# The masks' limits made two tiles at a time, and low parts moved ahead of them, in a fused attention and MLP kernel

## What is computed

```python
scores = scale * np.matmul(q, k.transpose(0, 1, 3, 2))        # 4 batches x 8 heads, 576 x 576, head_dim 64
thresh = np.max(scores, axis=-1, keepdims=True) - tau         # tau = 0.02
scores = np.where(scores >= thresh, scores, -1000000000.0)
attn = np.exp(scores - max); attn = attn / (sum + 1e-9); attn @ v
x = heads side by side                                        # 2304 tokens x 512
h = x @ w_in;  g = s * relu(h)**2 + b;  x = g @ w_out         # d_ff 2048
h = x @ w_in2; g = h * sigmoid(1.702 * h); out = g @ w_out2
```

## Time and profile before

| what | us |
|---|---|
| median of 3 runs (lowest to highest) | 1013.93 (1013.07 to 1015.03) |
| the profiled execution | 1013.14 |
| its span | 1011.3 |
| TensorE busy / VectorE busy | 988.5 (98%) / 796.9 (79%) |
| ScalarE / GpSimd busy | 606.3 (60%) / 658.3 (65%) |
| granted TensorE clock | full speed (1.00) throughout |

### The profile page before, as it was taken

One profiled execution on the slowest core, in us unless ns is written; L12 is line 12 of the kernel. 1 busy time (PEld: TensorE's weight loads), 2 busy tenths in 40 slices (PEclk: granted clock), 3 DMA queues, 4 the chain that ended last, 5 costly groups with the idle time before them and its releaser, 6 DMA issues.

```text
span 1011.3 us, 18111 instructions
## 1 busy us (share of the span) xinstructions
PE 988.5 (98%) x5872; PEld 890.6 (88%) x5872; DVE 796.9 (79%) x1747; ACT 606.3 (60%) x1124; POOL 658.3 (65%) x714
## 2 busy tenths in 40 slices
PE   5999999999999999999999999999999999999998
PEld 4888888888888888888899999998898989898897
DVE  6999999999999999999646765877667777556663
ACT  5887666666576666665545756554546545454453
POOL 5768997778888788887657775444534544445442
PEclk9999999999999999999999999999999999999999
DMA  6235776788777888678733441112122321222212
GB/s 205 82 99 168 204 207 208 193 242 237 211 192 196 225 218 222 191 185 214 207 122 126 172 162 34 41 64 84 42 84 71 118 84 43 83 82 106 84 47 78
DMA packets 97580, 142.48 MB, mean 141 GB/s; under 512 B 10320, under 2 KB 68944, under 8 KB 97488
## 3 DMA queue, kind: packets, MB, share of 16 engines
q1 hardware_dynamic: 97488, 141.34, 47.8%
HBM read 102.96 MB, written 4.72 MB: 106 GB/s over the span
## 4 chain that ended last, share of the span: by engine, by line
PE 87%; DVE 10%; issue 1%; ACT 1%; DMA 0%; POOL 0%; SPq 0%; DVEq 0%; POOLq 0%; ACTq 0%
PE shared L825 12%; PE y_ps L844 11%; PE shared L918 10%; PE y_ps L942 10%; PE scores L942 10%; PE scores L918 8%; PE scores L739 8%; PE scores L801 7%; PE scores L825 5%; PE y_ps L864 5%; DVE scores L1025 4%; DVE prob L1051 3%; PE scores L864 2%; DVE blocks L1065 1%; DVE limit L1032 1%
## 5 line engine op out<-in xcount | busy, mean ns | idle before, releaser
L1248 ACT ACTIVATE prob<-scores,neg_max 128x576 f32<-128x576 f32 (+1 forms) x160 | 118.6, 741 | 126.1 <-DVE scores L1025 124.0
L1590 POOL TENSOR_TENSOR a_sum_lo<-a_sum,a_hi 128x256 fp32r<-128x256 f32 x96 | 70.1, 740 | 182.7 <-DVE scores L1147 124.0
L1025 DVE TENSOR_SCALAR_CACHE_REDUCE scores<-scores,consts 128x576 f32<-128x576 f32 (+1 forms) x160 | 129.5, 809 | 18.1 <-PE scores L739 16.6
L1539 POOL TENSOR_TENSOR w_lo<-w_raw,win_hi 128x512 fp32r<-128x512 f32 x96 | 129.0, 1344 | 22.1 <-ACT win_hi L1290 17.7
L1546 POOL TENSOR_TENSOR w_lo<-w_raw,wout_hi 128x512 fp32r<-128x512 f32 x96 | 126.4, 1316 | 23.6 <-ACT wout_hi L1297 23.5
L1533 POOL TENSOR_SCALAR prob<-prob,row_inv 128x576 f32<-128x576 f32 (+1 forms) x160 | 126.5, 803 | 5.5 <-DVE row_inv L1039 5.0
L1051 DVE SCALAR_TENSOR_TENSOR prob<-scores,limit,prob 128x576 f32<-128x576 f32 (+1 forms) x160 | 128.1, 808 | 0.9 <-ACT act_hi L1258 0.9
L825 PE MATMUL shared<-act_hi,win_hi 128*128 128x384 f32 x280 | 94.9, 339 | 1.1 <-DVE gate L1081 0.9
L825 PE MATMUL shared<-act_hi,w_lo 128*128 128x384 f32 x280 | 94.4, 337 | 0.0
L739 PE MATMUL scores<-k_hi,q_hl 128*128 128x288 f32 (+1 forms) x320 | 78.0, 326 | 16.8 <-DVE prob L1051 9.0
L825 PE MATMUL shared<-act_lo,win_hi 128*128 128x384 f32 x280 | 94.0, 336 | 0.0
(11 more groups left out here) (154 smaller groups left out, 2945.1 us busy)
## 6 DMA issues: line engine op xcount, KB each, us to landing
w_raw<-slabs SPq DMA_DIRECT2D x93, 512.0 KB, 4.1
a_raw<-twin_in SPq DMA_DIRECT2D x24, 512.0 KB, 4.5
o_raw<-twin_out SPq DMA_DIRECT2D x24, 512.0 KB, 3.5
prob_t<-blocks SPq DMA_DIRECT2D x96, 120.0 KB, 2.7
k_raw<-k SPq DMA_DIRECT2D x32, 288.0 KB, 4.2
prob_t<-blocks SPq DMA_DIRECT2D x96, 96.0 KB, 2.9
v_sb<-v SPq DMA_DIRECT2D x26, 320.0 KB, 4.3
q_raw<-q SPq DMA_DIRECT2D x40, 192.0 KB, 4.4
```

What stands on the lines that cost most here:

```text
L1025: nc.vector.tensor_scalar(place, place, scale_c[0:m, :], None, ALU.mult, ALU.min, accum_out=neg_max[0:m, j % STATS:j % STATS + 1]).then_in ...
L1248: nc.scalar.activation(prob[0:m, j % PROBS, :].rearrange("p (a n) -> p a n", a=2), scores[j % 2][0:m, :, 0:HALF], ACT.Exp, bias=neg_max[0: ...
L1539: nc.gpsimd.tensor_tensor(in_of(w_lo, n), in_of(w_raw, n), win_hi[n % IN_HI][:].bitcast(F32), ALU.subtract).then_inc(win_lo_ready, 1)
```

## The change

The limits of both tiles of a beat become one instruction on two columns, which waits for both maxima (for `max_ready` at j + 2) and counts once for a pair, so that each mask waits for `limit_ready` at j // 2 + 1. It is issued after both maxima. The low part of the lone piece moves from between the two maxima to behind the second, and the low part of the gated slab from behind mask a to ahead of the limit.

```diff
-            def limit_of(j):
+            def limit_pair(j):
+
                 m, r = rows_of(j), j % STATS
-                dve.wait_ge(max_ready, j + 1)
-                nc.vector.tensor_scalar(limit[0:m, r:r + 1], neg_max[0:m, r:r + 1], tau_c[0:m, :], None, ALU.add
+                dve.wait_ge(max_ready, j + 2)
+                nc.vector.tensor_scalar(limit[0:m, r:r + 2], neg_max[0:m, r:r + 2], tau_c[0:m, :], None, ALU.add
                                         ).then_inc(limit_ready, 1)
...
-                dve.wait_ge(limit_ready, j + 1)
+                dve.wait_ge(limit_ready, j // 2 + 1)
...
                 for j in tiles_of(beat):
                     if j < TILES:
                         row_max(j)
-                        limit_of(j)
-                    if j % 2 == 0 and alone(beat - 1) is not None:
-                        context_lo(alone(beat - 1))
                     if j % 2 == 0 and 0 <= j - 2 < TILES:
                         invert_pair(j - 2)
                     if j % 2 == 0 and s >= 1:
                         gated(s - 1)
+                if alone(beat - 1) is not None:
+                    context_lo(alone(beat - 1))
+                if s >= 2:
+                    gated_lo(s - 2)
+                if 2 * beat < TILES:
+                    limit_pair(2 * beat)
                 for j in tiles_of(beat):
                     if j < TILES:
                         mask(j)
-                    if j % 2 == 0 and s >= 2:
-                        gated_lo(s - 2)
```

## The result

The changed kernel takes **1044.65 us** (median of 6 runs, 1041.83 to 1046.79) against 1014.36 (6 runs, 1013.07 to 1015.03): a ratio of 1.0296 [1.0282, 1.0309], some 30 us slower. Forecast were 1012.7 and a range to 1016.5.

A forecast was written before the change was run, and what follows sets the result against it. DVE and PE alternating bound early beats, DVE middle ones, PE late ones. Gains of 0.35 early and 1.3 middle, less 0.1 (beat 17) and 0.3 (late), made 1.25 us: 1013.93 to 1012.7, range 1010.2 to 1016.5.

The forecast's parts named there:

- The first rival: Early and middle beats: the pair's two-column limit also waits for POOL; about 9 us lost, 1023 us, chance 0.10.
- Early it gave 4.7 us: Early beats: the limit caught by POOL's second normalisation waits 0.48, losing 0.43 in each of 11 beats.
- 5.8 less 1.3: Middle: a caught limit loses 0.73 in each of eight beats, 5.8 us, less the forecast's 1.3 gain.
- DVE gets in between two of POOL's: Middle: DVE and POOL take turns by whole instruction, so the slab's low part lasts 0.94, not 0.61, in a normalisation.
- the forecast's own case: Early beats: 2.28 to 2.30 us against 2.35 from maximum a to mask a; 0.35 gained; whole case chance 0.50.
- the low part 0.20, which PE no longer covers: Early beats: the lone piece's low part, now behind maximum b, adds its 0.20 us on DVE ahead of the limit.
- the third one: Late: the slab's low part waits so long that PE stalls for masks; up to 10 us, about 1018, chance 0.15.
- Middle, the forecast's case: Middle beats 17 to 25: removed gaps partly paid, POOL hindering the slab's low part; 1.3 us gained of a possible 2.5.
- the 0.1 of beat 17: Start of the middle: the slab's low part meets a POOL weight split in that beat; 0.1 us lost.
- Late, the forecast's case: Late beats 26 to 79: change hidden behind PE, except waits for masks; 0.3 us lost.
- The gap behind a read: DVE: an independent instruction starts 0.03 us after a maximum's accumulator read, between bounds of 0 and 0.18.
- limit shows durations near 0.7: Sign that the forecast is wrong and the pair's limit is caught by POOL; the forecast expected 0.21 to 0.22.

The follow-up runs named there:

- e3: Kernel before, each of the 160 limits computed on two columns (its own and an unused one), order and count unchanged; 1039.7 us, ratio 1.0248.
- e1: Changed kernel's order, with two one-column limits in place of the pair's limit; 1016.89 us against 1014.78, ratio 1.0022.
- e8: Changed kernel, with POOL's q and k splits ahead of the normalisations in all beats; 1043.93 us in one run.
- e2: Changed kernel, pair's two-column limit kept behind the second maximum, both low parts back in their old places; 1022.11 us, ratio 1.0075.
- e5: Changed kernel with two one-column limits and the lone piece's low part back ahead of the second maximum; 1010.83 us against 1014.23, ratio 0.9968.
- e6: Kernel before, with only the lone piece's low part moved behind the second maximum and its limit; 1022.81 us, ratio 1.0086.
- e4: Kernel before, one-column limits put behind independent work, reciprocal and lone low part swapped; 1007.69 us against 1014.78, ratio 0.9932.
- e7: Changed kernel, the pair's limit made as a sum of two two-column tensors instead of tensor and scalar; 1017.88 us, ratio 1.0036.

## Why the prediction was wrong

**The first rival, given 0.10, is what happened; its size was a third of the real one.** The forecast costed the pair's limit at 0.21 of duration and took one-column limits (208 to 217 ns) and the two-column reciprocal (at most 158 ns) as evidence that such small operations slip past POOL. Neither row was of this kind with two columns, as the text said itself, and the weight on them was the mistake: e3 changes nothing but the width and loses 25 us, e1 takes the second column back and regains 28. A bound that no row of the same kind and width supports should have carried a chance nearer to a half than to a tenth, with a rule naming this very case beside it. The Trainium skill, "Vector Engine (DVE) Microarchitecture Reference", 5.1, has two elements per partition from one SBUF source run in a mode that takes both ports, and "SBUF — State Buffer", SBUF: two separate sides, has such an instruction and a GpSimd one exclude each other for a whole instruction. The traces agree for the one-source limit of two columns: 542 ns in the median, and its ends at 100.02 and 107.85 lie within 0.03 us of the end of a POOL instruction (99.99 and 107.83).

**The size of that rival.** Early it gave 4.7 us, from 0.43 in each of 11 beats. After minus e1, which differ in the width alone, is 1.0 early: the loop through PE hid most of it. In the middle it gave 5.8 less 1.3; after minus e1 is 14.6. The mis-sized term is the wait of one beat, put at one normalisation, 0.73. It is the rest of the second normalisation and then the q and k splits, up to 2.9 over the undisturbed 0.21, since these splits become ready when the slab's low part ends, just ahead of the limit. "DVE gets in between two of POOL's" was the false step as a rule: at 96.94 the limit let two pass that came behind the one it met, though in twelve late beats it did get in between. e8, with the splits elsewhere, has a longest of 1.41, and e2, with the low part behind, of 0.85. Late it was priced at nothing; after minus e1 is 8.6. The 54 limits there take 31.5 us, 20 more than at 0.215. Most held ones wait 0.5 (0.72 less 0.22), which is all of the 0.4 to 0.6 us of cover ahead of PE, and the longest wait 1.5.

**Early, the forecast's own case failed too.** It said 0.05 gained a beat and "the low part 0.20, which PE no longer covers", and so costed the moved low part by its duration on DVE. It did not ask who waits for it. TensorE's next context does, and the move put it behind maximum b, which PE itself feeds. e1 has this without the caught limit: 4.44 us a beat, 0.39 over 4.05, and 4.4 us in the stage. e5 puts the low part back and has -0.5; e6 moves it alone and has +7.9. Of the 4.4, none was foreseen by a rival: the third one had a stall of PE by a low part, but in the late stage.

**Middle, the forecast's case was right in kind** where its premise holds: 1.2 gained, with the 0.1 of beat 17 taken off the 1.3, and 1.24 measured in e1. That the tenth fits too is luck: e5, with the same order there, gains 2.0 in its profiled execution. The slab's low parts of e1 between 78 and 139 us had these durations:

```profile
L1091 DVE SCALAR_TENSOR_TENSOR g_lo<-gate,consts,g_hi x9: 609/785/1252, 88.8 to 137.3; 128x384 fp32r<-128x384 f32 x9
```

The median is under the foretold 0.9 to 1.2, the longest within 1.3.

**Late, the forecast's case was short:** 0.3 lost was forecast, e1 lost 1.3, and e5 2.1 in a profiled execution 2.1 above its median.

**The gap behind a read** was put at 0.03; in after it is 0: a read of a maximum and the independent reciprocal behind it start together.

```profile
41.03 0.14 DVE L1025 DVE_READ_ACCUMULATOR scores<-scores,consts 128x1 f32 x1
41.03 0.16 DVE L1040 RECIPROCAL row_inv<-row_sum_eps 128x2 f32<-128x2 f32 x1
```

To fill that gap is what the reordering is for. No run has it alone, but the two kernels that fill it with limits of one column and keep the lone low part ahead of maximum b are faster than before: e5 by 3.4 us and e4 by 7.1. The sign to look for, "limit shows durations near 0.7", was the right one: it names the first rival at sight.

## What to carry to other kernels

Merging two small VectorE operations changes their width, and the width can decide whether they have to wait for GpSimd: where GpSimd is busy most of the time, keep such an operation on one column, or test the wider form by itself before the order is built on it. Fill the gap behind an accumulator read with an independent instruction rather than save an instruction. Before an operation is moved behind another on its engine, ask who waits for it on other engines, and whether the one that it is put behind is fed by that same waiter.

## What the runs showed of the hardware

- The limit, a `tensor_scalar` with one tensor in SBUF as its source, takes 215 to 3077 ns on 128x2 or 96x2 floats beside a busy POOL, and 192 to 220 on one column in all kernels that had it. A two-column reciprocal, also one-source, was never held up in the kernel before (119 to 158 ns).
- A waiting VectorE instruction can see more than one GpSimd instruction go by: 3.08 us across the end of a normalisation, a q split and a k split. It does not always: in e2 a limit from 100.31 to 101.01 ends between a weight split and a normalisation.
- A sum of two two-column tensors takes 145 to 150 ns in most cases right behind another two-input operation of VectorE, and up to 1.61 us in some; elsewhere it was held about as often as the limit of after (e7).
- TensorE's granted clock was 1.00 in every stretch read of before. In after it fell twice to 0.50, the level of 1.2 GHz, each time behind a gap in which PE waited for a mask that the limit had held: 2.01 us of idle before the scores at 124.00, and 1.74 before those at 154.83. Such a gap did not always bring a fall: ahead of 108.76 PE was idle for 1.75 us, and from 108 to 114 the granted clock is 1.00. Stretches of 2 us of after (PE, PEld, DVE, ACT and POOL busy, then the granted clock and what the DMA engines did):

```profile
122.00:124.00 2.00, 0.00 (x0) 0.00 (x1) 1.97 (x4) 2.00 (x5) 1.06 (x1) 1.00 0.55 115
124.00:126.00 2.00, 2.00 (x18) 1.60 (x20) 2.00 (x5) 0.07 (x1) 1.24 (x2) 0.90 0.64 195
126.00:128.00 2.00, 2.00 (x13) 1.29 (x10) 1.34 (x5) 0.74 (x1) 2.00 (x3) 0.50 1.01 336
...
156.00:158.00 2.00, 2.00 (x18) 1.39 (x14) 2.00 (x6) 0.34 (x1) 2.00 (x2) 0.58 0.88 309
```

The context of 20 products that meets the fall takes 2.67 us at 124.74, where one at the full clock takes 1.85. From the scores behind the gap to the first output product it is 4.41 us at 124.00 and 4.52 at 154.83, and 3.08 in before for the same products (318.59 to 321.67). So the lower clock costs PE about 2.8 us more, beyond the idle time of the two waits.

What stays open: what decides whether a held limit gets in between two of POOL's instructions (in after twelve let a second one pass, six of them in the middle beats; all twelve work on 96 rows, and no run takes that apart from their place in the beats); why the two-input form is mostly let through behind a slab's low part; why more limits meet POOL in the late stage of e8; and what, besides idle time and the clock, makes the late stage of after longer.
